# A routed expert kernel on one core: list scatters that wait for each other, and the router's steps moved two places later

## The reference

```python
kv = np.einsum('bhsd,bhse->bhde', k, v)              # 8 batches, 8 heads, 576 tokens, head size 64
o = np.einsum('bhsd,bhde->bhse', q, kv)
x = o / np.sqrt(np.mean(o * o, -1, keepdims=True) + 1e-6) * g_norm     # then tokens x 512: 4608 rows
h = x @ w_in                                          # 512 -> 2048
y = (np.maximum(h, 0) + alpha * np.minimum(h, 0)) @ w_out              # -> 512
logits = y @ w_gate
e = argmax(logits, 1)                                 # one expert of 8 for each token
gate = softmax(logits)[n, e] * sigmoid((y @ w_output_gate)[n, e])
out[n] = gate * (np.maximum(y[n] @ w1[e], 0) @ w2[e]) # 512 -> 1024 -> 512
```

## Time and profile before

| | |
|---|---|
| median of 3 runs | 1532.9 us |
| lowest and highest | 1526.62, 1536.03 us |
| the profiled execution | 1532.9 us |
| its span in the trace | 1531.1 us |
| PE busy | 1493.1 us (98%) |
| DVE, ACT, POOL busy | 718.1, 503.4, 123.9 us |
| mean granted clock of PE | 0.989 |

### The profile page before, as it was taken

One profiled execution on the slowest core, in us unless ns is written; L12 is line 12 of the kernel. 1 busy time (PEld: TensorE's weight loads), 2 busy tenths in 40 slices (PEclk: granted clock), 3 DMA queues, 4 the chain that ended last, 5 costly groups with the idle time before them and its releaser, 6 DMA issues.

```text
span 1531.1 us, 28178 instructions
## 1 busy us (share of the span) xinstructions
PE 1493.1 (98%) x8061; PEld 1319.0 (86%) x8062; DVE 718.1 (47%) x1781; ACT 503.4 (33%) x1003; POOL 123.9 (8%) x139
## 2 busy tenths in 40 slices
PE   5999999999999999999999999998999999999997
PEld 5989999998999998999999999977888888888886
DVE  2685555564545454555556564664123114444411
ACT  3443232323232322223232322234233224444422
POOL 0000000000000000000000000111111111111111
PEclk8999999999999999999999999999999999999999
DMA  9332121102112101212110000444114114444410
GB/s 190 104 118 73 33 73 33 42 2 75 33 49 56 36 8 30 53 26 73 32 42 2 21 2 21 98 127 145 50 48 140 42 42 146 152 147 148 149 48 31
DMA packets 132023, 104.69 MB, mean 68 GB/s; under 512 B 92928, under 2 KB 107408, under 8 KB 131922
## 3 DMA queue, kind: packets, MB, share of 16 engines
q1 hardware_dynamic: 124050, 82.32, 19.3%
q0 software_dynamic: 7872, 21.09, 4.4%
HBM read 84.04 MB, written 20.65 MB: 68 GB/s over the span
## 4 chain that ended last, share of the span: by engine, by line
PE 93%; DMA 2%; DVE 1%; ACT 1%; SPq 1%; issue 1%; POOL 0%; POOLq 0%; ACTq 0%
PE psH L1262 26%; PE psAcc L1274 25%; PE psAcc L1386 14%; PE psH L1365 14%; PE psO L1192 3%; PE psO L1219 2%; PE psO L1375 2%; PE psY L1243 2%; PE psQ L1346 1%; PE psQ L1205 1%; PE psY L1237 1%; PE psY L1229 1%; DMA AR<-rows,uid 1%; DMA lists<-meta,slot 1%; DMA AR<-in_v_dram 0%
## 5 line engine op out<-in xcount | busy, mean ns | idle before, releaser
L1262 PE MATMUL psH<-XG,W 128*128 (+1 forms) x2304 | 441.8, 340 | 6.6 <-issue 4.0
L1274 PE MATMUL psAcc<-W,XG 128*128 128x512 f32 x1728 | 437.4, 398 | 0.0
L1262 PEld LDWEIGHTS psH<-XG,W 128*128 128x128 f32 x2304 | 413.4, 190 | 22.5 <-issue 5.0
L1274 PEld LDWEIGHTS psAcc<-W,XG 128*128 128x128 f32 x1728 | 314.3, 188 | 58.5 <-DVE XG L941 0.2
L652 ACT ACTIVATE XG<-AR 128x128 fp32r<-128x128 f32 (+1 forms) x384 | 138.0, 364 | 645.4 <-DVE AR L937 640.1
L934 DVE TENSOR_SCALAR AR<-psH,acol 128x384 f32<-128x384 f32 x192 | 118.6, 618 | 325.0 <-PE psH L1262 322.6
L1365 PE MATMUL psH<-W,XG 128*128 (+1 forms) x996 | 250.4, 400 | 1.1 <-DVE W L914 1.1
L1386 PE MATMUL psAcc<-W,XG 128*128 (+1 forms) x984 | 244.1, 397 | 0.0
L1386 PEld LDWEIGHTS psAcc<-W,XG 128*128 128x128 f32 x984 | 183.4, 190 | 37.5
L1365 PEld LDWEIGHTS psH<-W,XG 128*128 128x128 f32 x996 | 180.9, 188 | 38.4 <-DVE W L914 1.5
L1098 DVE TENSOR_TENSOR XG<-psO,XG 128x512 fp32r<-128x512 f32 x82 | 56.6, 691 | 217.8 <-ACT XG L710 214.5
(11 more groups left out here) (175 smaller groups left out, 906.3 us busy)
## 6 DMA issues: line engine op xcount, KB each, us to landing
AR<-in_moe_w_dram SPq DMA_DIRECT2D x68, 512.0 KB, 5.5
AR<-in_k_dram SPq DMA_DIRECT2D x64, 144.0 KB, 3.2
AR<-in_v_dram SPq DMA_DIRECT2D x16, 576.0 KB, 5.4
rows<-AR SPq DMA_DIRECT2D x36, 256.0 KB, 2.1
AR<-in_q_dram SPq DMA_DIRECT2D x32, 256.0 KB, 3.1
AR<-in_moe_w_in_dram SPq DMA_DIRECT2D x16, 256.0 KB, 2.9
AR<-in_moe_w_out_dram SPq DMA_DIRECT2D x16, 256.0 KB, 3.1
AR<-in_q_dram SPq DMA_DIRECT2D x8, 128.0 KB, 3.2
```

The lines of the kernel that those rows point to most:

```text
L1262: mm = pe.matmul(psH[f % 2][:, 0:TILE], w_in_v[:, wp, cc, f * P:(f + 1) * P], xT[:, b, xp, cc, :], start=(cc == 0 and (wp, xp) == PARTS[0] ...
L1274: mm = pe.matmul(psAcc[m][:, :], gT[:, f % 2, gp, m * P:(m + 1) * P], w_out_v[:, wp, f, :], start=(f == 0 and (gp, wp) == PARTS[0]), stop= ...
```

## The change

Three parts.

- **One semaphore for the lists.** `listed0` to `listed2` become one, `listed`, and each scatter waits for the landing of the one ahead before it is issued. DVE and SP wait for the one semaphore at three times the count, at the same places.
- **The router two steps later.** In each tile, y transposes and logits go from steps 1 to 6 to steps 3 to 8, pick from 7 to 9, exps from 8 to 10, ranks and place from 9 to 11. In the last tile choose_star goes from 9 to 11, the splits of pieces 0 and 1 from steps 12 and 13 to 13 and 14.
- **The first unit behind the tile.** x_units(0) goes from step 15 to behind the last tile, h_unit(0, 0) behind the first of the y transposes. ACT splits unit 0's rows behind pieces 2 and 3 and the first y_evacuate, DVE behind pieces 2 and 3.

```diff
-        listed = [sem(f"listed{m}") for m in range(TG)]
+        listed = sem("listed")
@@ SP, behind the tiles; the same for 16 * TG * TILES further on
-            for m in range(TG):
-                sp.wait_ge(listed[m], 16 * (TILES - 1))
+            sp.wait_ge(listed, 16 * TG * (TILES - 1))
             load_ids(0, 0)
@@ POOL, put_in_lists(t)
                 for m in range(TG):
                     pool.indirect_dma_start(lists, bass.IndirectOffsetOnAxis(ap=slot[:, m:m + 1], axis=0),
-                                            meta[:, m, 1:2].bitcast(I32), None).then_inc(listed[m], 16)
-                for m in range(TG):
-                    pool.wait_ge(listed[m], 16 * t + 16)
+                                            meta[:, m, 1:2].bitcast(I32), None).then_inc(listed, 16)
+                    pool.wait_ge(listed, 16 * TG * t + 16 * m + 16)
                     pool.sem_inc(pool_passed, 1)
@@ ACT, tile
-                    if before and f == 8:
+                    if before and f == 10:
                         exps(t - 1)
-                    if not ahead and f in (12, 13):
-                        expert_high(0, f - 12)
+                    if not ahead and f in (13, 14):
+                        expert_high(0, f - 13)
@@ ACT, behind the tiles
-            ux(0)
             for n in (2, 3):
                 expert_high(0, n)
             y_evacuate(TILES - 1, 0)
+            ux(0)
             y_evacuate(TILES - 1, 1)
@@ DVE, tile
-                    if before and f in (1, 3, 5):
-                        yT_copy(t - 1, (f - 1) // 2)
-                    if before and f in (2, 4, 6):
-                        lg_copy(t - 1, (f - 2) // 2)
+                    if before and f in (3, 5, 7):
+                        yT_copy(t - 1, (f - 3) // 2)
+                    if before and f in (4, 6, 8):
+                        lg_copy(t - 1, (f - 4) // 2)
-                    if before and f == 7:
+                    if before and f == 9:
                         pick(t - 1)
-                    if before and f == 9:
+                    if before and f == 11:
                         place(t - 1)
-                    if not ahead and f == 9:
+                    if not ahead and f == 11:
                         choose_star()
-                    if not ahead and f in (12, 13):
-                        expert_low(0, f - 12)
+                    if not ahead and f in (13, 14):
+                        expert_low(0, f - 13)
                 if before:
                     dve.wait_ge(meta_saved, 16 * t)
-                    for m in range(TG):
-                        dve.wait_ge(listed[m], 16 * t)
+                    dve.wait_ge(listed, 48 * t)
@@ DVE, behind the tiles
-            ux(0, 0, 0)
             for n in (2, 3):
                 expert_low(0, n)
+            ux(0, 0, 0)
@@ PE, side(s)
-                    if before and s in (1, 3, 5):
-                        y_transpose(t - 1, (s - 1) // 2)
-                    if before and s in (2, 4, 6):
-                        logits(t - 1, (s - 2) // 2)
+                    if before and s in (3, 5, 7):
+                        y_transpose(t - 1, (s - 3) // 2)
+                    if before and s in (4, 6, 8):
+                        logits(t - 1, (s - 4) // 2)
-                    if before and s == 9:
+                    if before and s == 11:
                         ranks(t - 1)
-                    if not ahead and s == 15:
-                        x_units(0, 0, 0)
@@ PE, behind the tiles
-            h_unit(0, 0)
+            x_units(0, 0, 0)
             for m in range(TG):
+                if m == 1:
+                    h_unit(0, 0)
                 pe.wait_ge(y_set, 3 * t + m + 4)
```

More of the change, by code:

```diff
@@ L436, in _ @@
             sp.wait_ge(tab_set, 1)
-            for m in range(TG):
-                sp.wait_ge(listed[m], 16 * TILES)
+            sp.wait_ge(listed, 16 * TG * TILES)
             next_ids(2, 0, 1)
```

## The result

The changed kernel takes 1545.1 us (median of 4 runs, 1544.0 to 1546.2) where the kernel before takes 1531.2 (median of 4): a ratio of 1.0096, with a 95% interval from 1.0074 to 1.0117. That is 0.96% slower, clear of zero, and its interval lies on both sides of the 1% line of the forecast. The forecast was 1549.7 us, 1.1% slower, with a range of 1535 to 1565; it was reckoned from 1532.9 us, the median of the first three runs of the kernel before.

A forecast was written before the change was run, and what follows sets the result against it. TensorE (PE), busy 98% of 1531.1 us, was taken as the bound, so only its waits count. Hand-over 6.0, unit 3 5.6 and clock 5.2 sum to 16.8 us on 1532.9: 1549.7 us, +1.1%, range 1535 to 1565.

The forecast's parts named there:

- Bound and direction: PE is busy 98% of 1531.1 us, so only its waits can change the time; slower, +1.1%.
- signs of being wrong: Wrong if a lone scatter is under 3.8 or over 5.5 us, gather much over 4.2, or PE waits inside tiles.
- Rival 4: Not slower: lone scatters of 2.0 us make the series 7.6 us, under 9.5; about 1533 us; chance 0.11 with the rest.
- Part 1: In the token tiles, the router's move of two steps (8.7 us) costs 0; delayed star expert work is costed at nothing.
- Part 2: List scatters in series: 4.5 us each and 0.8 between, 15.1 us in place of 9.5, 5.6 more.
- The tile ends: DVE's wait for lists at each tile's end: 20.5 to 22.4 us left, the 15.1 us series fits, cost 0.
- Rival 3: Scatters above 7.1 us make PE wait at the end of ten tiles; at 8 us about 1586 us; chance 0.05.
- Part 3: Hand-over to the units: PE waits 5.9 us for unit 0's rows, h_unit(0,0) starts 6.0 us later.
- part 5: Half clock behind each of the two new waits for rows costs 2.6 us, 5.2 us in all.
- rival 2: Scatters of 6 to 7 us, 1559 us at 6.1, or a gather of 8.5 under load, 1554; chance 0.12.
- Part 4: At x_units(3), the last three lists in series delay unit 3's gather: + 5.6 us.
- Unit 4 "unchanged": The 4.34 us wait at unit 4 hangs on the table behind x_units(3), moves with it and stays the same.

The follow-up runs named there:

- e2: The kernel before with only the three list scatters in series, all else as before; 1539.5 us, ratio 1.0047.
- e3: The kernel before with only the router moved two steps later, scatters together, x_units(0) in step 15; 1540.3 us, ratio 1.0058.
- e1: The changed kernel with the three list scatters issued together again, each with its own semaphore; 1536.6 us, ratio 1.0040 to the kernel before.
- e10: The changed kernel run once more unaltered, beside the one with the hold on pieces 4 to 7; 1548.8 us, ratio 1.0109 to the kernel before.
- e5: The changed kernel with the star expert's pieces 4 to 7 issued only after unit 0's gather has landed; 1543.8 us, ratio 1.0087 to the kernel before.
- e11: The changed kernel with the star expert's pieces 4 to 7 held until unit 0's gather landed, run again; 1543.0 us, ratio 1.0082 to the kernel before.
- e7: The kernel before with only the last tile's three list scatters in series; 1532.2 us, +0.13%, ratio 1.0013.
- e6: The kernel before with the second expert's pieces 4 to 7 issued only after unit 4's gather has landed; 1533.1 us, ratio 1.0022.
- e8: The kernel before with only the second expert's pieces 6 and 7 held until unit 4's gather has landed; 1528.6 us, ratio 0.9994.
- e4: The kernel before with only x_units(0), ux(0) and h_unit(0,0) in their later places; 1531.2 us, ratio 1.0000.
- e9: The changed kernel with scatters together and the splits of star pieces 0 and 1 in steps 14 and 15; 1536.7 us, ratio 1.0030 to the kernel before.
- e12: The changed kernel with scatters together, row numbers read only after star pieces 0 to 3 have landed; 1540.3 us, ratio 1.0060 to the kernel before.

## Why the prediction was right, and where not

**Bound and direction: right.** PE's work is unchanged, and the loss is PE's waiting for gathered rows. e2 and e3 each bring about half of it by itself (0.47 and 0.58 points of 0.96), so both the series and the move carry it. The list of PE's waits was forecast at about 17 us in three and has 16.7 in three, but that is luck: the parts were to be 5.9, 6.6 and 4.3 and are 10.7, 3.2 and 2.8. And one of my own signs of being wrong came true, the gather that lands much later than 4.2 us (7.0). Rival 4, the not-slower one, gave a lone scatter 2.0 us, as the Trainium skill (DMA: Bandwidth & Descriptors, section "Anatomy of one DMA — SWDGE (gpsimd) path") has it for so few bytes. The trace disagrees: 2.5 us at the least, 4.2 on the median. The measurement decides. (The rival's break-even was mis-reckoned, too: the series equals 9.5 us at (9.5 - 1.6) / 3 = 2.63 us a scatter, not 2.55.)

**Part 1, two steps later at no cost in the tiles: right for PE's work, wrong for the cover in the last tile.** The first ten moved tiles show no wait of PE beside those at the loop's ends that were there before. But the sentence "what they delay is over before the gather below, so I cost them at nothing" failed as a rule: in e1 the late star pieces gave a wait of 3.48 us. In the change itself they cost 0.79 us, because there the pieces landed in 5.2 us, and that was hidden behind the late rows. So the term was near zero in the sum for another reason than mine.

**Part 2, the length of the series: right on the whole, wrong as one number.** Forecast 4.5 us a scatter and 0.8 between; measured 4.2 (median) and 0.8 (a landing at 981.91, the next start at 982.71). But the two series that matter were not alike. At the hand-over it took 975.86 to 993.03, 17.2 us and not 15.1; at unit 3 from 1032.24 to 1043.6, 11.4.

**The tile ends: right.** In the ten tiles with another behind them the longest series was 17.5 us (from 826.88 to 844.4), under the 20.5 that I had counted as free, and PE's list has no wait there. Rival 3 did not happen. In the last tile, which is shorter, DVE did wait 0.69 us for the lists (2.23 in e10), at its split of piece 2; PE was waiting for the rows by then.

**Part 3, the hand-over: right chain, too small, the term that was mis-sized most.** Forecast + 6.0, and with half of part 5 + 8.6; measured 12.8 to h_unit(0,0) and 2.0 behind it. This is the term of the sum that failed. From the 5.9 us of PE's wait to the 10.7 measured: + 2.1 for the series, + 1.3 for the way from SP's issue to the gather (993.77 to 997.92, 4.2 and not 2.9), + 2.8 for the gather (7.0 and not 4.2), - 0.8 for the wait of PE just ahead of it, and the rest, - 0.6, since the first scatter stood that much earlier against the end of the last matmuls. The gather's part is shown by e5 and e11: without the pieces beside it, 3.4 us. I had written of just this danger under rival 2 and not put it in the main sum.

**Part 4, unit 3: right place, too large.** Forecast + 5.6, measured + 2.3: the last tile's three scatters, with little else in flight, took 3.3 us each on the mean. Against the 9.99 us from first scatter to gather stand 1044.65 - 1032.24 = 12.4. e7 shows the term by itself.

**Unit 4 "unchanged": wrong by 2.6 us to the good.** Its wait fell from 4.34 to 2.79, its gather took 6.5 us in place of 8.5, and the half clock behind it was shorter. e7 gives back 1.9 us at the same place, so most of this seems to come with the series at unit 3; why the gather is quicker then, no experiment tells.

**Part 5, the clock: right.** Forecast 2 x 2.6; measured 2.7 behind unit 3, and 2.4 in h_unit(0,0), which took 5.46 us and not 3.02. The stretch from its start to x_units(2) shows only 2.0 of it, since one group of transposes now stands ahead of it. A few tenths more are inside the 12.8: from x_units(0) to h_unit(0,0) it took 2.6 us and not 2.0. The stretches after (us, PE busy, granted clock, DMA share, GB/s) show the fall behind the long wait and the return:

```profile
995.00:999.00 4.00, 0.00 (x0) 1.00 0.24 45
999.00:1003.00 4.00, 0.00 (x0) 0.53 0.93 301
1003.00:1007.00 4.00, 1.97 (x8) 0.50 0.98 374
1007.00:1013.00 6.00, 5.45 (x14) 0.51 0.26 91
1013.00:1018.00 5.00, 5.00 (x42) 1.00 0.39 118
```

0.50 is the 1.2 GHz level and 1.00 the 2.4 GHz level; PE had done nothing for several microseconds when it fell. The DMA share of 0.98 in the third row is the traffic that the gather had to share.

**The 3.0 us that the last tile came sooner** I had not forecast, and it is not the change's. In the profile of before the clock fell to half at two ends of the tile loop, after about 2 us without a matmul (1.86 and 2.15; each row has busy time and count of PE, PEld, DVE, ACT and POOL, then the granted clock, the DMA share and GB/s):

```profile
361.00:364.00 3.00, 3.00 (x10) 3.00 (x11) 0.00 (x0) 0.54 (x2) 0.00 (x0) 0.51 0.56 205
607.00:610.00 3.00, 3.00 (x13) 2.91 (x12) 0.92 (x3) 0.00 (x0) 0.00 (x0) 0.50 0.42 154
```

In the first profile of the change it did not (2.03 and 1.80 us without a matmul; the hidden block behind took 2.35 and 2.37 us, where before it took 3.91 and 3.30); in e10, the same kernel, it did at both (3.90 and 3.32). In e2, which has no move, it did at neither. Single profiles differ by this, a little over 3 us in all, and by several us more in the start (the first of these blocks starts at 358.22 in e1 and at 364.39 in e10). e6, e7 and e8 are the kernel before up to the last tile, and there their last hidden blocks start at 985.94, 985.41 and 989.34, where the profile of before has 989.77.

**The sum** came out 2.9 us above the measured increase of 13.9 because errors of both signs met. With the clock's part in each, the hand-over was forecast at 8.6 and measured at 14.8, too low by 6.2; unit 3 at 8.2 and measured at 5.0, too high by 3.2; unit 4 too high by 2.6; and the last tile came 3.0 sooner in the profile, the end 0.4. That the forecast is close is in good part luck, and doesn't make its parts exact. The other 1.7 us between 1549.7 and 1545.1 are the start value: 1532.9 in three runs, 1531.2 in four.

## What to carry to other kernels

Give each DMA in flight its own semaphore rather than a wait ahead of the next: the Trainium skill (DMA: Bandwidth & Descriptors, section "Why a DMA increments its semaphore by 16 and not by 1") says so for safety, and here the one shared semaphore, with the waits that it needs, cost about 0.5% (0.47 in e2, 0.56 from e1 to the change) though POOL has little else to do; no run here shows the hazard itself. At a hand-over between two phases, follow the whole chain of small DMAs from the last result to the first matmul, and look at what is issued close to each of them: four loads of 512 KB doubled the time of a gather (3.4 us without, 7.0 and 8.0 with). And don't price a wait at its length on the profile without following the next ones: e7's longer wait at unit 3 was in part given back at unit 4, and of the 4.1 us that e6 won at unit 4 the next three units took back 3.1.

## What the runs showed of the hardware that was not expected

Three scatters of 128 four-byte words in flight together slow the large loads issued next. The four pieces of 512 KB for the star expert took, from issue to landing on the median: with the scatters together 9.2 (before), 10.0 (e1), 9.9 (e3), 9.9 (e4), 9.4 (e6), 9.2 (e7), 9.2 (e8), 10.3 (e9) and 9.7 us (e12); in series 5.2 (the change), 6.0 (e2), 5.1 (e5), 5.6 (e10) and 5.7 us (e11). The line for the kernel before, and for the change:

```profile
DMA to landing us min/median/max: 9.2/9.2/9.2
```

```profile
DMA to landing us min/median/max: 5.0/5.2/5.4
```

The loads are not slowed evenly: they start late. The stretches below have the columns of those in part 5 above. SP issues the pieces from 974 in the kernel before:

```profile
975.00:977.00 2.00, 2.00 (x11) 1.00 0.56 8
977.00:979.00 2.00, 2.00 (x13) 1.00 0.68 57
979.00:981.00 2.00, 2.00 (x11) 1.00 0.75 55
981.00:983.00 2.00, 2.00 (x13) 1.00 0.99 399
```

and from 979 in the change:

```profile
980.00:982.00 2.00, 2.00 (x12) 1.00 1.10 66
982.00:984.00 2.00, 2.00 (x12) 1.00 0.77 317
984.00:986.00 2.00, 2.00 (x12) 1.00 1.03 420
```

Before, next to nothing moves for 7 us, until 981, 1 us behind the third scatter's landing (972.98 + 7.0 = 980.0); from then on the rate is that of the change, where the slow start lasts 3 us. In e1, e4 and e12 it lasts 7 to 8 us, in e2, e10 and e11 about 4.

So the series has a good side, which the kernel before could not use: there the splits of these pieces stand late enough. A lone scatter of 512 bytes took from 2.5 to 6.7 us in one and the same kernel. What sets it isn't shown; the same scatter takes much the same in another kernel (the first of three in the ninth, eleventh and twelfth lists: 6.7, 6.0 and 2.5 us in the change, 7.0, 6.6 and 2.5 in e2).
